# Reading the moving rows of every matrix product from the last token of a block to the first

## The reference

```python
sig = 1.0 / (1.0 + np.exp(-f_logit))
f = lower_bound + (1.0 - lower_bound) * sig
for t in range(S):                      # S = 6080, two sequences, 256 channels
    h = f[:, t] * h + (1.0 - f[:, t]) * x[:, t]
    y[:, t] = h
x = y.reshape(B * S, D)                 # 12160 tokens of 256 channels
h = x @ w_in                            # 256 -> 2048
g = np.where(h > 0.0, h, np.exp(np.minimum(h, 0.0)) - 1.0)
out = g @ w_out                         # 2048 -> 256
```

## Time and profile before

| what | value |
|---|---|
| median of three runs | 990.57 us |
| the profiled execution | 990.41 us |
| its span, first to last instruction | 988.6 us |
| TensorE busy | 982.2 us, 4362 matmuls |
| weight loads busy | 817.1 us |
| ScalarE, VectorE, GpSimd busy | 793.0, 728.0, 631.9 us |

### The profile page before, as it was taken

How to read it: one execution, slowest core, us unless ns; L and a number is a source line. 1 busy time by engine, 2 the same in 40 slices (tenths; PEclk the granted TensorE clock), 3 DMA queues, 4 the chain that set the end, 5 groups by cost and what they waited for, 6 DMA issues and landing times.

```text
span 988.6 us, 15352 instructions
## 1 busy us (share of the span) xinstructions
PE 982.2 (99%) x4362; PEld 817.1 (83%) x4362; DVE 728.0 (74%) x915; ACT 793.0 (80%) x1425; POOL 631.9 (64%) x474
## 2 busy tenths in 40 slices
PE   8999999999999999999999999999999999999998
PEld 5888888888888888888888888888888888888997
DVE  6896876886786697688679668758867957875544
ACT  7988878878887887888788788788788788778775
POOL 2686887567657557656755855765675675576454
PEclk9999999999999999999999999999999999999999
DMA  7102002101201100210210120021021012000001
GB/s 277 64 23 74 33 1 76 54 1 53 74 0 42 53 32 0 74 53 0 64 64 0 42 64 21 21 55 52 0 71 56 0 46 70 0 0 13 33 1 38
DMA packets 23211, 41.88 MB, mean 42 GB/s; under 512 B 2704, under 2 KB 4240, under 8 KB 23184
## 3 DMA queue, kind: packets, MB, share of 16 engines
q1 hardware_dynamic: 22752, 41.04, 12.8%
q10 hardware_dynamic: 432, 0.53, 0.2%
HBM read 29.10 MB, written 12.45 MB: 42 GB/s over the span
## 4 chain that ended last, share of the span: by engine, by line
PE 99%; DMA 1%; DVE 0%; ACTq 0%; ACT 0%; issue 0%
PE acc L866 17%; PE acc L864 17%; PE acc L865 17%; PE h L838 14%; PE h L840 14%; PE h L836 14%; PE h L961 1%; PE h L959 1%; PE h L960 1%; DMA x<-value 1%; PE h L940 0%; DVE x L603 0%; PE h L931 0%; PE acc L961 0%; PE acc L959 0%; PE acc L940 0%
## 5 line engine op out<-in xcount | busy, mean ns | idle before, releaser
L317 POOL TENSOR_TENSOR g_lo<-e,g_hi 128x512 fp32r<-128x512 f32 (+1 forms) x384 | 519.4, 1362 | 351.0 <-ACT g_hi L458 349.5
L444 ACT ACTIVATE e<-h 128x512 f32<-128x512 f32 (+1 forms) x380 | 226.0, 595 | 151.4 <-PE h L840 129.3
L694 DVE SCALAR_TENSOR_TENSOR e<-e,h 128x512 f32<-128x512 f32 (+1 forms) x380 | 256.8, 676 | 70.3 <-ACT e L450 70.0
L866 PE MATMUL acc<-g_hi,w_out_lo 128*128 128x512 f32 (+1 forms) x768 | 297.3, 387 | 0.0
L864 PE MATMUL acc<-g_hi,w_out_hi 128*128 128x512 f32 (+1 forms) x768 | 297.3, 387 | 0.0
L865 PE MATMUL acc<-g_lo,w_out_hi 128*128 128x512 f32 (+1 forms) x768 | 297.2, 387 | 0.0
L450 ACT ACTIVATE e<-e 128x512 f32<-128x512 f32 (+1 forms) x384 | 241.5, 629 | 8.4
L458 ACT CAST g_hi<-e 128x512 fp32r<-128x512 f32 (+1 forms) x384 | 232.4, 605 | 16.9 <-DVE e L694 16.9
L838 PE MATMUL h<-a_lo,w_in_hi 128*128 128x512 f32 (+1 forms) x616 | 238.4, 387 | 0.0
L836 PE MATMUL h<-a_hi,w_in_hi 128*128 128x512 f32 (+1 forms) x616 | 238.2, 387 | 0.0
L840 PE MATMUL h<-a_hi,w_in_lo 128*128 128x512 f32 (+1 forms) x616 | 238.2, 387 | 0.0
(11 more groups left out here) (72 smaller groups left out, 564.6 us busy)
## 6 DMA issues: line engine op xcount, KB each, us to landing
out<-out_sb SPq DMA_DIRECT2D x44, 256.0 KB, 2.0
gate<-forget_logit SPq DMA_DIRECT2D x43, 256.0 KB, 2.6
x<-value SPq DMA_DIRECT2D x43, 256.0 KB, 2.7
w_in_raw<-w_in SPq DMA_DIRECT2D x8, 256.0 KB, 6.2
w_out_raw<-w_out SPq DMA_DIRECT2D x8, 256.0 KB, 7.1
x<-value SPq DMA_DIRECT2D x4, 224.0 KB, 2.5
gate<-forget_logit SPq DMA_DIRECT2D x4, 224.0 KB, 2.5
out<-out_sb SPq DMA_DIRECT2D x4, 224.0 KB, 1.9
```

Source lines behind the costliest of these rows:

```text
L317: nc.gpsimd.tensor_tensor(g_lo[:, t % RING, 0:w], e[:, t % TILES, 0:w], g_hi[:, t % RING, 0:w].bitcast(F32), ALU.subtract).then_inc(g_lo_r ...
L444: nc.scalar.activation(e[:, i, 0:w], bank_of(j, t)[:, 0:w], ACT.Relu, scale=-1.0).then_inc(r_ready, 1)
L694: nc.vector.scalar_tensor_tensor(e[:, t % TILES, 0:w], e[:, t % TILES, 0:w], -1.0, bank_of(j, t)[:, 0:w], ALU.add, ALU.max).then_inc(g_rea ...
L866: done = nc.tensor.matmul(bank, lo, g_hi[:, t % RING, 0:w], start=False, stop=closes)
```

## The change

In every product the moving operand is sliced with a step of -1 along the tokens. So the array gets the last token of the block first, and the column that it writes first in the PSUM tile belongs to the last token. The hidden tile lies in PSUM from the last token to the first, the ELU and the combinations between tiles work on it in that order, and `g_hi` and `g_lo` hold it so. The second layer reads these with a step of -1 again, and the output in `acc` stands in the order of tokens as before. The sums are the same, element by element.

The number of instructions on each engine, their order, their shapes and their waits are the same in both programs; on TensorE only the line numbers differ. What differs is the access pattern of the moving operand in 4344 of TensorE's 4362 matmuls. The PSUM side of the matmuls, and all operands of the other engines, are read and written forward as before.

```diff
+            def backward(part):
+
+                return part[:, ::-1]
+
             def product(j, par, q, k, bank, start=False):
                 w = width(j)
                 hi, lo = w_in_hi[:, q, k], w_in_lo[:, q, k]
-                a_h, a_l = a_parts(par, k)
-                nc.tensor.matmul(bank[:, 0:w], hi, a_h[:, 0:w], start=start, stop=False,
+                a_h, a_l = [backward(part[:, 0:w]) for part in a_parts(par, k)]
+                nc.tensor.matmul(bank[:, 0:w], hi, a_h, start=start, stop=False,
                                  skip_group_check=True)
-                nc.tensor.matmul(bank[:, 0:w], hi, a_l[:, 0:w], start=False, stop=False,
+                nc.tensor.matmul(bank[:, 0:w], hi, a_l, start=False, stop=False,
                                  skip_group_check=True)
-                return nc.tensor.matmul(bank[:, 0:w], lo, a_h[:, 0:w], start=False, stop=True,
+                return nc.tensor.matmul(bank[:, 0:w], lo, a_h, start=False, stop=True,
                                         skip_group_check=True)
...
                 bank = acc[:, b, half, 0:w]
-                nc.tensor.matmul(bank, hi, g_hi[:, t % RING, 0:w], start=opens, stop=False)
-                nc.tensor.matmul(bank, hi, g_lo[:, t % RING, 0:w], start=False, stop=False)
-                done = nc.tensor.matmul(bank, lo, g_hi[:, t % RING, 0:w], start=False, stop=closes)
+                g_h, g_l = backward(g_hi[:, t % RING, 0:w]), backward(g_lo[:, t % RING, 0:w])
+                nc.tensor.matmul(bank, hi, g_h, start=opens, stop=False)
+                nc.tensor.matmul(bank, hi, g_l, start=False, stop=False)
+                done = nc.tensor.matmul(bank, lo, g_h, start=False, stop=closes)
...
-                pieces = [a_parts(0, PLACE[0][i]) for i in range(HALVES)]
+                pieces = [[backward(part) for part in a_parts(0, PLACE[0][i])] for i in range(HALVES)]
...
-                    a_h, a_l = a_parts(0, PLACE[b][half])
+                    a_h, a_l = [backward(part) for part in a_parts(0, PLACE[b][half])]
```

## The result

The changed kernel takes 1018.38 us (median of four runs, 1018.23 to 1019.29) beside 990.56 us for the kernel before on the same chip: 27.8 us more, a ratio of 1.0282 with a 95% interval of 1.0264 to 1.0299. It is slower. Its profiled execution has a span of 1016.4 us.

What follows compares the result with a forecast made beforehand. TensorE's matmul count times its pace was taken to bound the kernel: 976.2 us plus 14.2 us of edges. All terms of the change were 0, so 990.41 + 0, on the median 990.6 us; range 988 to 1107.

Steps and rivals of the forecast that it cites:

- likeliest case: TensorE's moving reads: pace per matmul unchanged within 0.46 ns either way, so 990.6 us; chance 0.64.
- rival B: Fixed toll at each TensorE matmul's start; the 13.3 ns gap once more 58 us, twice more 116 us; chance 0.14.
- What bounds the kernel: TensorE: the number of matmuls times their pace sets the run's length, with everything else hidden under it.
- Step 1: ELU steps reading whole product tiles: they wait for the last matmul in either order; term 0.
- Step 2: Backward moving reads in TensorE's matmuls: 4344 times the change in pace d, with d taken as 0; term 0.
- Step 3: Weight loads beside the matmul ahead: 39 ns of cover at 512 columns, about 15 at 448; taken as 0.
- 188 plus 15: 448-column matmuls: their pace of 202.8 ns read as about a weight load, 188 ns, plus 15.
- A: Array's fetch of moving rows: half pace, each column its own fetch, 440 ns per matmul, 1906 us; chance 0.14.
- C: Moving reads on TensorE: columns slower by the weight loads' ratio of 1.61, 555 us more, 1546 us; chance 0.04.
- D: Moving reads on TensorE: pace of the weight loads, 1.47 ns per column, 3305 us; chance 0.02.
- E: Gap of 13.3 ns per TensorE matmul: some of it goes, at most 53 us faster, 937 us; chance 0.02.
- pair rule: VectorE's port streams fully only on aligned adjacent pairs; applied to moving reads, columns take 1.64 times as long, about 1577 us.

Runs made afterwards that it cites:

- first set of series: The kernel before with 24 series of 60 matmuls each put ahead of the first product; at 512 columns forward 226.7 ns, backward 233.3 ns.

## Why the prediction was right in part and wrong in its likeliest case

The measured 1018.4 lies inside the range, but the likeliest case, no change with a chance of 0.64, was wrong. That the range holds it is in part luck: its upper end was set by rival B, and B's mechanism is not what the runs show.

- *What bounds the kernel.* Right: TensorE's pace times its matmuls, with nothing to hide a slower one. The 27.8 us are 4344 matmuls at the new pace, and no wait changed hands.
- *Step 1, the readers.* Right: no cost and no gain. The kernel that writes PSUM backward has the same order at 990.68.
- *Step 2, the moving reads.* This step failed. It took d = 0 because the new matmul was "nearest" to the old one in its words and columns; d is 6.7 ns at 512 columns and 3.9 at 448. It treated the gap of 13.3 ns as something between matmuls that the change does not alter. The runs show that the gap depends on the order of the 16-byte groups and on where rows and weights lie: at 512 columns it runs from 5.4 ns (one word 512 times) over 13.3 (forward, in place) and 20 (backward, or forward out of place) to 26.7 (backward from word 514), and bf16 has 2.5.
- *Step 3, the weight loads.* Their cover of 39 ns was no answer. The loads kept 188 ns and, after the change, still ended 41 ns before the next matmul's start on average, so by the cover nothing should have happened; and the bound of "188 plus 15" read from the 448 columns was wrong, since 432 columns go at 195.7 ns.
- *Rival B* had the sign and the form (some ns in each matmul), and neither the size nor the mechanism: its smaller price was the whole gap once more, 58 us, and the runs show half of that. A toll at each start is refuted by the step of 2, by 384 columns, and by a forward kernel that pays the same after a shift of 32 bytes. *A, C, D and E* did not occur.
- *Two prices of rivals* were misread. C's ratio of 1.61 set loads of bf16 weights that ran partly at the lower clock (117 ns on average) beside fp32r ones at the upper; in the first set of series bf16 loads take 97 to 98 ns, which makes the ratio 1.9. D's 1.47 ns per column spread a fixed part over the columns: loads of 2, 32, 64, 96 and 128 columns take 83, 108, 134, 161 and 188 ns, about 0.83 ns for each further column. Neither changes which case came true.

On the two rules weighed: "Advanced Engine Details and Errata" of the Trainium skill, section "SBUF Cachelines", asks for two accesses in a row to the same 16-byte line. That words reversed inside a group of four are free (226.7 ns) agrees with a line of that size. But a step of 2 floats, two words of each line, took 451 ns, and pairs of adjacent words 453.8, so for moving rows in fp32r two words of a line are not enough here; and which way the lines go counts, on which the section has nothing. The pair rule of the Trainium skill's "Vector Engine (DVE) Microarchitecture Reference", section 5.2, did not carry over: a backward read costs the array 3%, not the 64% estimated from it.

Shown: the cost is tied to the order of the 16-byte groups and to where rows and weights lie to one another, once and not twice. Open: what in the memory or in the array makes the one place favourable, why a start 4 words off breaks the rule of the distance, why forward reads in place lose 2 to 5 ns with fewer weight columns, and why a backward read finds no such place at any of the starts tried. That the weight load itself is what the read of the rows collides with is not shown: every matmul of the series loads its own weights, so no run shows the pace without a load beside it. No start tried gave less than 226 ns at 512 columns with rows read in full, so no version beats both kernels; the one that has the ELU's order without the cost is the write to PSUM in reverse, at the time of before.

## What to carry to other kernels

In a kernel that is all matmuls, a few ns in the pace are the whole story, and the pace between starts is worth comparing at once in ticks: 544 against 560. Where an order must be reversed, reverse it on the PSUM side or in VectorE's copy out, both free here, and not in fp32r moving rows. In fp32r matmuls of 512 columns with 128 weight columns, let the moving rows begin on a multiple of 32 bytes and keep their distance from the weights in SBUF a multiple of 256 bytes: every such place tried kept 226.7 ns. Check it when a small tensor is added in between.

## What the hardware showed that was not expected

- 32 bytes of allocation ahead of the moving rows cost 27.5 us (ratio 1.0278), as much as the whole change.
- A change of direction between matmuls costs on its own, about 20 ns there and back: 18.5 us for backward reads in the first layer, where 13.1 were worked out for its matmuls alone.
- Moving rows of fp32r with a step of 2 go at half the pace, 451 ns for 512 columns.
- VectorE's copy out of PSUM took 684 ns backward where it took 685 forward.
